# Products of probabilities and v, the two heads of a pair alternating matmul by matmul

## The reference

```python
def _attn_ref(q, k, v, n_sink, window):          # 2 batches, 8 heads, 768 positions, 64 per head
    scores = (1.0 / np.sqrt(D)) * np.matmul(q, k.transpose(0, 1, 3, 2))
    keep = is_sink | in_window                    # 4 sink columns, a causal window of 128
    scores = np.where(keep, scores, -1000000000.0)
    scores = scores - np.max(scores, axis=-1, keepdims=True)
    a = np.exp(scores)
    a = a / (np.sum(a, axis=-1, keepdims=True) + 1e-09)
    return np.matmul(a, v).astype(np.float32)     # the product that the change touches
...
x = attention output as 1536 tokens x 512
x = _moe_ref(x, w_in, w_out, g_ln)                # h = x @ w_in, SoLU, layer norm, @ w_out
return _moe2_ref(x, w_gate, w1, w2)               # 8 experts of 512-1024-512, all run on all tokens,
                                                  # weighted by a gate normalised 8 times
```

## Time and profile before

| what | us |
|---|---|
| median of three timed runs | 1378.34 (1374.97 to 1379.07) |
| the profiled execution | 1376.82 |
| its span | 1375.0 |
| loop passes of stage A, from the first turn of head 1's probabilities to the last such turn | 30.18 to 144.79 |
| last scores, last pair and first projections | 144.79 to 177 |
| the rest of stages B and C | 177 to 1375 |

### The profile page before, as it was taken

The page is one execution under the profiler, slowest core; times in us unless marked ns, Lnnn a source line. Parts: engine busy times, 40 slices in busy tenths (PEclk is TensorE's granted clock), DMA queues, the critical chain, the costliest instruction groups (busy, mean ns, idle before and its releaser), DMA issues.

```text
span 1375.0 us, 16253 instructions
## 1 busy us (share of the span) xinstructions
PE 1335.9 (97%) x6103; PEld 1091.8 (79%) x6103; DVE 500.2 (36%) x964; ACT 261.5 (19%) x555; POOL 319.8 (23%) x179
## 2 busy tenths in 40 slices
PE   5888999998999999999999999999999999999999
PEld 5656678876888888888888888888888888888887
DVE  6888553435522222323222222222222223232322
ACT  5655543421110101010202010101011010101020
POOL 6555021133011111111222221111111111111110
PEclk9988999999999999999999999999999999999999
DMA  5443100001000000000000001100000000000002
GB/s 166 145 140 99 64 0 1 1 31 61 0 31 31 31 31 31 31 31 31 31 31 31 31 32 41 48 31 31 31 31 31 31 31 31 31 31 31 31 0 92
DMA packets 15988, 56.94 MB, mean 41 GB/s; under 512 B 2144, under 2 KB 4192, under 8 KB 11872
## 3 DMA queue, kind: packets, MB, share of 16 engines
q1 hardware_dynamic: 14848, 55.28, 11.5%
q10 hardware_dynamic: 1120, 1.39, 0.3%
HBM read 53.51 MB, written 3.15 MB: 41 GB/s over the span
## 4 chain that ended last, share of the span: by engine, by line
PE 91%; DVE 5%; issue 2%; ACT 1%; DMA 0%; DVEq 0%; ACTq 0%; SPq 0%
PE ps L493 28%; PE ps L495 28%; PE ps L494 28%; PE ps L473 2%; DVE probs L931 2%; PE ps L436 2%; PE ps L407 1%; PE ps L578 1%; DVE probs L908 1%; PE ps L408 1%; PE ps L482 1%; DVE acc L1040 0%; ACT acc L814 0%; PE ps L412 0%; DVE gate L1130 0%
## 5 line engine op out<-in xcount | busy, mean ns | idle before, releaser
L493 PE MATMUL ps<-w_unit,h_hi 128*128 128x512 f32 x768 | 298.9, 389 | 0.0
L495 PE MATMUL ps<-w_unit,h_lo 128*128 128x512 f32 x768 | 298.8, 389 | 0.0
L494 PE MATMUL ps<-w_unit,h_hi 128*128 128x512 f32 x768 | 298.8, 389 | 0.0
L886 ACT ACTIVATE h_hi<-ps 128x512 fp32r<-128x512 f32 x192 | 114.9, 598 | 908.7 <-PE ps L495 908.7
L493 PE MATMUL ps<-x_hi,w_unit 128*128 128x512 f32 x720 | 280.1, 389 | 0.0
L494 PE MATMUL ps<-x_lo,w_unit 128*128 128x512 f32 x720 | 280.1, 389 | 0.0
L495 PE MATMUL ps<-x_hi,w_unit 128*128 128x512 f32 x720 | 280.1, 389 | 0.0
L1184 DVE SCALAR_TENSOR_TENSOR acc<-ps,gate_now,acc 128x512 f32<-128x512 f32 x192 | 144.2, 751 | 355.5 <-PE ps L495 355.5
L1109 DVE SCALAR_TENSOR_TENSOR h_lo<-ps,h_hi 128x512 fp32r<-128x512 f32 x192 | 132.8, 692 | 385.5 <-ACT h_hi L886 385.5
L373 POOL TENSOR_SCALAR w_unit<-w_raw 128x2048 fp32r<-128x2048 f32 x31 | 59.5, 1919 | 813.6 <-PE ps L495 808.4
L493 PEld LDWEIGHTS ps<-w_unit,h_hi 128*128 128x128 f32 x768 | 144.1, 188 | 30.0
(11 more groups left out here) (129 smaller groups left out, 1108.6 us busy)
## 6 DMA issues: line engine op xcount, KB each, us to landing
w_raw<-w_exp SPq DMA_DIRECT2D x32, 1024.0 KB, 4.8
q_raw<-qT SPq DMA_DIRECT2D x16, 384.0 KB, 4.3
k_raw<-kT SPq DMA_DIRECT2D x16, 384.0 KB, 4.0
out<-acc SPq DMA_DIRECT2D x12, 256.0 KB, 2.0
w_raw<-w_in SPq DMA_DIRECT2D x8, 256.0 KB, 2.7
w_raw<-w_out SPq DMA_DIRECT2D x8, 256.0 KB, 2.9
v_sb<-v SPq DMA_DIRECT2D x9, 192.0 KB, 3.6
v_sb<-v ACTq DMA_DIRECT2D x7, 192.0 KB, 2.4
```

What stands on the lines that cost most here:

```text
L493: pe.matmul(o, ws[0], xs[0], start=first, stop=False)
L494: pe.matmul(o, ws[0], xs[1], start=False, stop=False)
L495: return pe.matmul(o, ws[1], xs[0], start=False, stop=last)
L886: act.activation(h_hi[:, g, :], bank(g % 4), ACT.Relu).then_inc(h_hi_out, 1)
```

## The change

`pv(p, g)` now does one group of both heads: m = g and m = g + 3. For each v block and span of query tiles it issues the matmul of head 0 and right behind it that of head 1. So there are three blocks of pv for a pair, of 6, 4 and 4 matmuls, in place of six blocks. They stand after step 8, after step 10, and in step 0 of the pass after; step 1 keeps only the sinks. Each block waits for the PSUM copies of both heads' groups, and the first for both loads of v. `va_used` is raised by the third block, which is in step 0 of the pass after instead of step 10. For the last pair the three blocks and the turns stand anew between the projections. Matmuls, operands and waits of everything else are as before.

```diff
-            def pv(p, m):
+            def pv(p, g):
-                h, n0, n1 = t_group(m)
...
-                if m % 3 == 0:
-                    pe.wait_ge(v_loaded[h], 16 * p + 16)
-                if m == 0:
+                for m in (g, g + 3):
...
+                if g == 0:
+                    pe.wait_ge(v_loaded[0], 16 * p + 16)
+                    pe.wait_ge(v_loaded[1], 16 * p + 16)
                     pe.wait_ge(x_out, p + 1)
-                rows_h = slice(64 * h, 64 * h + 64)
+                n0, n1 = t_group(g)[1:]
                 for j in range(n0 // 2, (n1 + 1) // 2):
...
                     for t0, t1 in spans:
...
-                        last = pe.matmul(o, vj, pT[:, h, n * P:(n + t1 - t0) * P],
+                        for h in range(2):
+                            rows_h = slice(64 * h, 64 * h + 64)
...
+                            last = pe.matmul(o, v_sb[:, h, j * DH:(j + 1) * DH],
+                                             pT[:, h, n * P:(n + t1 - t0) * P],
...
-                if m == 2:
+                if g == 2:
                     last.then_inc(va_used, 1)
             def end_of_pair(p, k):
                 if k == 0:
-                    pv(p, 4)
+                    pv(p, 2)
                 if k == 1:
-                    pv(p, 5)
                     pv_sinks(p)
-            PV_AFTER = {7: 0, 8: 1, 10: 2, 11: 3}
+            PV_AFTER = {8: 0, 10: 1}
...
             h1_half(0, 0)
             turn(last_pair, 2)
-            pv(last_pair, 0)
-            pv(last_pair, 1)
             turn(last_pair, 3)
             turn_sinks(last_pair)
             h1_half(0, 1)
+            turn(last_pair, 4)
+            pv(last_pair, 0)
+            h1_half(1, 0)
+            turn(last_pair, 5)
+            pv(last_pair, 1)
+            h1_half(1, 1)
             pv(last_pair, 2)
-            turn(last_pair, 4)
-            h1_half(1, 0)
-            pv(last_pair, 3)
-            turn(last_pair, 5)
-            h1_half(1, 1)
-            pv(last_pair, 4)
-            pv(last_pair, 5)
             pv_sinks(last_pair)
```

More of the change, by code:

```diff
@@ L445, in turn_sinks @@
                 last.then_inc(sinkT_full, 1)
-            def pv(p, m):
-                h, n0, n1 = t_group(m)
[L450 to L455, removed]
-                if m % 3 == 0:
-                    pe.wait_ge(v_loaded[h], 16 * p + 16)
-                if m == 0:
+            def pv(p, g):
+                for m in (g, g + 3):
+                    if m in PT_ON_ACT:
+                        n = len(PT_ON_ACT)
+                        pe.wait_ge(pT_act, n * p + (n + PT_ON_ACT.index(m) + 1))
+                    else:
+                        n = len(PT_ON_DVE)
+                        pe.wait_ge(pT_dve, n * p + (n + PT_ON_DVE.index(m) + 1))
+                if g == 0:
+                    pe.wait_ge(v_loaded[0], 16 * p + 16)
+                    pe.wait_ge(v_loaded[1], 16 * p + 16)
                     pe.wait_ge(x_out, p + 1)
-                rows_h = slice(64 * h, 64 * h + 64)
+                n0, n1 = t_group(g)[1:]
                 for j in range(n0 // 2, (n1 + 1) // 2):
-                    vj = v_sb[:, h, j * DH:(j + 1) * DH]
                     spans = [(j, min(j + 2, QT))]
@@ L467, in pv @@
                     for t0, t1 in spans:
[L468 to L471, removed]
                         n = 2 * j + (t0 - j)
-                        last = pe.matmul(o, vj, pT[:, h, n * P:(n + t1 - t0) * P],
-                                         start=(j, t0) in ((0, 0), (1, 2)), stop=False,
-                                         skip_group_check=True)
-                if m == 2:
+                        for h in range(2):
+                            rows_h = slice(64 * h, 64 * h + 64)
+                            if t0 < 2:
+                                o = bank(X_BANK)[rows_h, t0 * P:t1 * P]
+                            else:
+                                o = bank(X_BANK + 1)[rows_h, (t0 - 2) * P:(t1 - 2) * P]
+                            last = pe.matmul(o, v_sb[:, h, j * DH:(j + 1) * DH],
+                                             pT[:, h, n * P:(n + t1 - t0) * P],
+                                             start=(j, t0) in ((0, 0), (1, 2)), stop=False,
+                                             skip_group_check=True)
+                if g == 2:
                     last.then_inc(va_used, 1)
```

## The result

The changed kernel takes 1365.28 us (median of four runs, 1365.01 to 1365.81). The kernel before, with the run that was made beside it, has a median of 1378.70 (1374.97 to 1385.89, four runs). The ratio is 0.9908, interval 0.988 to 0.9936: about 0.9% faster, and the forecast was 1366.5. The profiled execution took 1365.01 us with a span of 1363.2, so the two profiled spans differ by 11.8 us.

What follows compares the result with a forecast made beforehand. PE and DVE were taken as nearly level in the loop, PE as full behind it. Savings of 6.0 + 2.4 + 3.5 = 11.9 us from 1376.8 gave 1364.9, plus 1.5 for the median: 1366.5; own range 1360 to 1371, overall 1359 to 1378.

Steps and rivals of the forecast that it cites:

- Block cost and overlap: Products on PE: 0.25 us fixed per block, 0.213 a unit; heads overlap fully, so a pair takes 3.4 us, 2.8 less.
- The chain in a pass: In a loop pass: POOL starts 0.8 us later, +8.2; step 0 near +8.5, not +10.4; step 1's scores read about +14.0.
- The wait that I said would go: Second half of a pass: DVE's 1.04 us wait for PE's scores of step 2 disappears.
- Loop, 6.0 us from the passes: Six loop passes: about 17.2 of 18.16 us stay, 1.0 saved a pass, 6 in all; bounds 0 and 2.0 a pass.
- The clock, 2.4 us saved: Loop passes: of 5.4 us lost to the low clock, 3.0 stay; bounds 5.4 saved and 3.5 for each further pass.
- rival 3: Loop: faster PE waits more, clock falls each pass, costing 3.5 us; 1384.4; sign: clocks 0.8 and below in four passes; chance 0.09.
- Behind the loop, 3.5 us: From the last pass to the last sinks, PE full: two pairs' shorter products save 3.5 us; bounds 5.1 and 1.0.
- the upper bound of 5.1: Behind the loop: the most that could be saved, two pairs' products at 2.8 and 2.3 us.
- the wait on the weight segment: Behind the loop: first projection waits for a weight segment through ACT and DVE, one reason for taking 3.5 of 5.1 us.
- v of head 0 asked for later: Loop loads: v requested in step 0, not step 10, about 3 us later, q and k queued behind; costed at nothing.
- Rival 1: Products in loop and behind: no overlap, 5.44 us of PE a pair; only 3 us gained, 1375.3; chance 0.22.
- Rival 2: Product blocks: loads of v no longer hide when the head changes, 14 x 0.137 us; 5 us slower, 1383; chance 0.12.

Runs made afterwards that it cites:

- the last experiment: Changed kernel with its second block behind step 11's scores, not step 10's, plus three idle-time matmuls in each of three places: 1374.51 us, ratio 0.9971.

## Why the prediction was right

Step by step, as it was put:

- **Block cost and overlap: right.** 0.25 us around a block and 0.213 a unit gave 1.88, 1.87 and 1.44 in the kernel without overlap, and full overlap is what the starts show. The blocks are even a little shorter than I had, 1.02 for "1.1 to 1.3".
- **The chain in a pass: right, each step somewhat late.** POOL at +8.42 for +8.2, step 0 at +8.83 for +8.5, step 1's scores read at +14.31 for +14.0; in the pass from 101.53 POOL starts at +8.79, where PE did more of that half at the low clock (its block of twelve took 1.38 us to the next start for 1.02). The wait that I said would go is gone. That POOL's end sets this was only argued from rows then; with POOL's subtraction cut, DVE's two instructions beside it take 0.54 us again.
- **Loop, 6.0 us from the passes: too small.** Full-clock passes took 17.10 us, as forecast (17.2), but those of the kernel before take 18.5, not the 18.2 I had averaged from passes of unlike clocks; the earlier trace rows had one of 18.52 at full clock. Five passes, the second to the sixth, took 85.49 us with filling matmuls and 92.49 in the kernel before with them: 7.0 us, 1.4 a pass for the 1.0 I had. The first pass can't be compared so: each kernel begins it at the low clock, and for how long differs (its second turned blocks took 0.66 us at 34.18 in the kernel before, 0.90 at 34.56 in the filled one), which alone makes it 18.66 us there for 17.77.
- **The clock, 2.4 us saved: the step that failed.** Against the filled kernels the low clock cost 96.84 - 92.49 = 4.35 us in these five passes before and costs 89.34 - 85.49 = 3.85 now: 0.5 saved. In the first pass, 0.4 us longer than before, the clock now falls once as well, so that about nothing is left of the 2.4. The premise of rival 3 came true, the clock falls in every pass, and so did the sign that I had named for it, four passes at 0.8 and below; its price did not: about 0.8 us a pass for the 3.5 I had. That the rest lies in PE's slack is my reading, not shown by itself.
- **Behind the loop, 3.5 us: 3.53 measured.** The number is luck, the reason was wrong: at full clock it is 32.14 - 27.49 = 4.65, near the upper bound of 5.1, and what took 1.1 of it away is the low clock in that stretch (0.94), not the wait on the weight segment that I gave as reason.
- **v of head 0 asked for later: no cost**, as said. In the pass shown PE waits for ACT's copies (0.36 and 0.63 us), not for a load, and in the passes of that profile neither PE nor POOL waits for one.
- **Rival 1** was mis-sized: without overlap the kernel takes 1379.3, not 1375.3; its clock falls in every pass, which the rival did not price, but what that costs there was not measured. **Rival 2** (loads of v exposed when the head changes) is excluded by the same kernel, whose alternating units in one half still take 0.213 us.

So 11.8 us came out where 11.9 was summed, and that it is so close is luck. The mechanism (overlap, fewer blocks, a shorter pass) was right, but the loop had two errors of opposite sign, the passes priced too low and the clock too high. Together the two terms are 8.4 us, and the six passes brought 7.06, 1.3 less; 0.68 + 0.53 = 1.2 us from ahead of the passes and behind the sinks, which the sum had not priced, made up for it.

## What to carry to other kernels

Where two fp32 matmuls load 64 columns each (the only size tried here), put their results in different partition halves and issue them as neighbours; near is enough, strict alternation cost nothing to leave out for runs of four records a head, and 0.48 us a block for runs of six. Price a faster PE by what its end starts: here the last score of a half starts POOL and POOL holds up DVE. Step 0 began 1.57 us sooner, yet step 1's scores were read 0.41 us later than before; what the pass gained is the wait of 1.04 us behind them that went. Where PE waits in a loop, read the clock by pass, and try filling the waits with work that nobody reads before looking for finer orders; 5.1 us came of it here. Filling that runs past the end of the wait delays the engine, as in the last experiment.

## What the runs showed of the hardware

- Two fp32 matmuls with 64 loaded columns each, in different column halves, run at the same time in full: 22 units of a pair in the time of 11, starts 7 ns apart, each with a loaded v of its own. In one half they don't at all.
- Matmul records started out of program order: head 1's first (159.058 us) started ahead of head 0's fourth (159.162). The Trainium skill, "TensorE: Matmul & The Clock Gate", The mechanism, says that matmuls start and end in program order and that a load overlaps a running matmul only where the row group differs. The first doesn't agree with the starts above; nor does the second with two loads and two matmuls over the same 128 rows that take 0.44 us together.
- The granted clock fell to 1.2 GHz once in each pass of the changed kernel, after waits of 1.0 to 1.6 us close together, and stayed at 2.4 GHz in all passes with four matmuls of 0.43 us more. In the kernel before it fell twice in the loop, each time after a wait of 2.2 us.
- A POOL subtraction of 1.81 us makes DVE's 0.35 us normalising last until it ends (1.63 us; two of 128 columns took 2.10 for 0.54). The Trainium skill, "SBUF — State Buffer", Who interferes with whom, tells of a port pair that the two share and of which the one that comes second waits in full; the rows agree, and with the subtraction cut to 16 columns a pass is 2.2 us shorter.
